# Second projection as one run of 36 matmuls behind the seven products, and the gates' sums over tokens on TensorE

## The chip, the cores and the metric

The kernel runs on one core of a Trainium2 chip. The metric is the device time of one execution in microseconds (us), lower is better. Engines are named PE (TensorE), DVE (VectorE), ACT (ScalarE), POOL (GpSimd) and SP (the queue that starts the loads); PEld is the load of PE's stationary operand.

## The reference

Chunked attention (2 x 8 heads, 768 tokens, head size 64) is followed by two mixtures of experts over 1536 tokens of 512 numbers: one with 4 experts and given gates, one with 8 experts whose gates are worked out from the first one's output by eight rounds of dividing by row sums and by column sums.

```python
def _moe_ref(x, domain_probs, w1, w2):
    p = domain_probs / (domain_probs.sum(-1, keepdims=True) + 1e-09)
    for e in range(E):                       # 4 experts
        h = np.maximum(x @ w1[e], 0.0)       # w1[e]: 512 x 1024
        out += p[:, e:e + 1] * (h @ w2[e])   # w2[e]: 1024 x 512

def _moe2_ref(x, w_gate, w1, w2):
    logits = x @ w_gate                      # 1536 x 8
    P = np.exp(logits - logits.max())
    for _ in range(8):
        P /= P.sum(1, keepdims=True) + 1e-09
        P /= P.sum(0, keepdims=True) + 1e-09  # over all 1536 tokens
        P *= N / E
    for e in range(E):                       # 8 experts
        out += P[:, e:e + 1] * (np.maximum(x @ w1[e], 0.0) @ w2[e])
```

## The kernel before

After the attention (the first 110 us) the work is 96 equal steps that the code calls quads: 24 jobs (an expert for one half of the tokens, 768) of four quads. The jobs stand in four passes of 4, 4, 8 and 8 jobs, so a new set of token operands begins at quads 16, 32 and 64 (called boundaries below). Every product of two fp32 matrices is made of three matmuls in the fp32r type, on a rounded high part and a low part that holds the rest (`in_three`, L438 to L441).

**First projection.** A quad makes four 128x384 blocks of the hidden layer from seven products (Winograd's form of a 2x2 block product). Product i (L443) is six matmuls of 384 columns. It accumulates in one of four PSUM banks, in the order `CHAIN = (0, 1, 0, 3, 0, 2, 3)`: products 2, 4 and 6 go on top of what is in a bank that ACT has first to copy away. So product 2 waits for `keep_part` 0, product 4 for `keep_part` 1 and product 6 for `keep_part` 2 (L453 to L460, L625). DVE then adds the kept parts to each block (`add`, L763), ACT makes the rounded hidden value (`hidden`, L630) and DVE its low part (`hidden`, L770).

**Second projection.** `down` (L467) multiplies two finished quads (a half of the hidden layer) by half of w2, for six token tiles; a tile is twelve matmuls of 512 columns. Quad q runs three tiles of the half before it, in twelve pieces of three matmuls that stand between the products as `PIECES = (2, 2, 1, 2, 2, 2, 1)` says. The first piece of an even quad waits for all hidden blocks of the quad just before it (L471). DVE adds a finished tile to the output rows (`accumulate`, L776).

**Weights.** SP loads w1 for a quad once `w1_raw` is free, which is when DVE's low part of the quad before is done (L245, `split_s` L747). POOL forms four sums (`sum_s`, L304), ACT rounds all seven stationary operands (`split_s`, L606), DVE takes the low part. w2 is rounded on ACT (L612) and its low part taken on DVE (`split_w2`, L752).

**Boundaries.** In the last quad of a pass ACT and DVE also make the seven token operands of the next pass (`next_tokens`, `split_t`, L618 and L758), and POOL forms sums of them (`sum_t` L314, `sum_t4` L334).

**Gates.** After the first mixture the output rows are transposed on PE (`turn_rows`, quads 18 and 33 to 34) and multiplied by `w_gate` (`logits`). From quad `SINK0` = 35 on DVE runs the eight rounds, three to a quad (`gates`, L820): row sums on DVE alone, column sums by DVE over a partition's tokens, then over the 128 partitions by POOL's `partition_all_reduce`. In POOL's queue these stand behind `sum_s(quad + 2)`:

```python
if quad + 2 < ALLQ:
    sum_s(quad + 2)
...
if SINK0 <= quad < SINK0 + 3:
    for it in range(3 * (quad - SINK0), min(3 * (quad - SINK0) + 3, SINKHORN)):
        pool.wait_ge(csum_ready, it + 1)
        pool.partition_all_reduce(ctotal, csum, P, RED.add).then_inc(ctotal_ready, 1)
```

No engine's queue is reordered: what stands behind a waiting instruction in the program text of its engine waits too.

## Time and profile before

| | |
|---|---|
| time, median of 3 runs | 1722.59 us (1720.34 to 1725.53) |
| profiled execution: its time | 1730.89 us |
| profiled execution: span | 1729.1 us |
| mean granted TensorE clock | 0.963 |
| PE busy | 1626.9 us, 94% of the span |
| DVE busy | 1003.6 us, 58% |
| ACT busy | 690.9 us, 40% |
| POOL busy | 329.8 us, 19% |

The span runs from the first to the last instruction of the profiled execution. PE's busy share counts overlapping matmuls as one, so how fast PE goes is read from the starts of successive matmuls. A granted clock of 1 is the full 2.4 GHz, 0.5 is the lower level of 1.2 GHz.

### The profile page before, as it was taken

Reading aid. Unit: us, or ns where it says so; the run is one execution under the profiler, and the core shown is the slowest. Engines: PE = TensorE matmul, PEld = TensorE weight load, DVE = VectorE, ACT = ScalarE, POOL = GpSimd, SP = SyncE. Lnnn points to the kernel's source line nnn. Section 1 sums busy time; section 2 is a strip of 40 time slices with the busy share of each in tenths; the row PEclk is TensorE's granted clock in tenths of the full one; section 3 lists DMA queues with packets and bytes.
Section 4 is the critical chain, followed back from the end, with each engine's and each line's share of the span. In section 5 each row is a group of like instructions: output and inputs, shape, how many; then the busy total and the mean of one; then the engine's idle time right before and its main releaser. Section 6 shows DMA issues by size and latency. Waiting matters only on the chain.

```text
span 1729.1 us, 21400 instructions
## 1 busy us (share of the span) xinstructions
PE 1626.9 (94%) x8673; PEld 1448.9 (84%) x8673; DVE 1003.6 (58%) x1445; ACT 690.9 (40%) x1058; POOL 329.8 (19%) x429
## 2 busy tenths in 40 slices
PE   6659999989999989759999999998999999999999
PEld 6648888879888879648888888887888888888887
DVE  5455655664565564536656565657565556556563
ACT  5443344443334443213444434434334443444441
POOL 2211113121111322011111111132111111111110
PEclk9779999999999999889999999999999999999999
DMA  9832122211212221111121222121222121121210
GB/s 161 127 67 85 62 62 72 62 49 49 86 61 62 73 61 49 40 46 49 61 73 62 61 86 62 49 85 49 97 85 61 50 86 61 56 79 62 78 57 37
DMA packets 158930, 117.75 MB, mean 68 GB/s; under 512 B 31336, under 2 KB 129640, under 8 KB 158832
## 3 DMA queue, kind: packets, MB, share of 16 engines
q1 hardware_dynamic: 158832, 116.39, 23.9%
q8 instruction: 68, 1.11, 0.3%
q14 instruction: 30, 0.25, 0.1%
HBM read 113.22 MB, written 3.15 MB: 67 GB/s over the span
## 4 chain that ended last, share of the span: by engine, by line
PE 85%; DVE 5%; SPq 3%; issue 2%; DMA 2%; ACT 1%; POOL 1%; POOLq 0%
PE banks L439 28%; PE banks L441 28%; PE banks L440 28%; SPq L229 1%; DVE t_lo L760 1%; DVE s_lo L749 1%; SPq L228 1%; DMA w_raw<-in_moe_w 1%; PE banks L497 1%; DVE banks L768 1%; ACT h_hi L632 1%; DMA v_bd<-in_mem_v 1%; DVE h_lo L772 1%; PE banks L425 0%; PE banks L489 0%
## 5 line engine op out<-in xcount | busy, mean ns | idle before, releaser
L439 PE MATMUL banks<-t_lo,s_hi 128*128 128x384 f32 x1344 | 459.6, 342 | 35.9 <-DVE h_lo L772 33.3
L439 PE MATMUL banks<-w_lo,h_hi 128*128 128x512 f32 x1152 | 459.7, 399 | 20.6 <-DVE h_lo L772 19.9
L440 PE MATMUL banks<-w_hi,h_hi 128*128 128x512 f32 x1152 | 459.5, 399 | 0.0
L441 PE MATMUL banks<-w_hi,h_lo 128*128 128x512 f32 x1152 | 458.7, 398 | 0.0
L441 PE MATMUL banks<-t_hi,s_lo 128*128 128x384 f32 x1344 | 456.9, 340 | 0.0
L440 PE MATMUL banks<-t_hi,s_hi 128*128 128x384 f32 x1344 | 454.5, 338 | 0.0
L768 DVE TENSOR_TENSOR banks<-banks,part 128x384 f32<-128x384 f32 x384 | 216.3, 563 | 362.7 <-PE banks L441 220.9
L632 ACT ACTIVATE h_hi<-banks 128x384 fp32r<-128x384 f32 x384 | 188.9, 492 | 555.3 <-DVE banks L768 555.3
L628 ACT ACTIVATE part<-banks 128x384 f32<-128x384 f32 x384 | 188.8, 492 | 392.8 <-PE banks L441 392.6
L439 PEld LDWEIGHTS banks<-t_lo,s_hi 128*128 128x128 f32 x1344 | 256.5, 191 | 67.1 <-issue 36.4
L772 DVE SCALAR_TENSOR_TENSOR h_lo<-banks,h_hi 128x384 fp32r<-128x384 f32 x384 | 213.4, 556 | 163.7 <-ACT h_hi L632 163.7
L307 POOL TENSOR_TENSOR w_raw<-w_raw 128x256 f32<-128x256 f32 x96 | 72.3, 753 | 1206.0 <-DMA w_raw<-in_moe_w 1206.0
L440 PEld LDWEIGHTS banks<-t_hi,s_hi 128*128 128x128 f32 x1344 | 256.1, 191 | 28.0
L439 PEld LDWEIGHTS banks<-w_lo,h_hi 128*128 128x128 f32 x1152 | 219.0, 190 | 59.3 <-DVE h_lo L772 35.8
L441 PEld LDWEIGHTS banks<-w_hi,h_lo 128*128 128x128 f32 x1152 | 218.5, 190 | 48.8
L441 PEld LDWEIGHTS banks<-t_hi,s_lo 128*128 128x128 f32 x1344 | 255.8, 190 | 0.0
L790 DVE SCALAR_TENSOR_TENSOR rows<-banks,gate,rows 128x512 f32<-128x512 f32 x258 | 192.3, 745 | 82.1 <-PE banks L441 82.1
L440 PEld LDWEIGHTS banks<-w_hi,h_hi 128*128 128x128 f32 x1152 | 218.8, 190 | 23.2
L749 DVE TENSOR_TENSOR s_lo<-w_raw,s_hi 128x1792 fp32r<-128x1792 f32 x96 | 193.5, 2016 | 0.0
L610 ACT ACTIVATE s_hi<-w_raw 128x1792 fp32r<-128x1792 f32 x96 | 162.6, 1694 | 2.1 <-POOL w_raw L312 2.1
L755 DVE TENSOR_TENSOR w_lo<-w_raw,w_hi 128x1024 fp32r<-128x1024 f32 x96 | 117.0, 1219 | 2.4 <-ACT w_hi L615 2.4
L615 ACT ACTIVATE w_hi<-w_raw 128x1024 fp32r<-128x1024 f32 x96 | 101.0, 1052 | 0.0
(87 smaller groups left out, 642.5 us busy)
## 6 DMA issues: line engine op xcount, KB each, us to landing
w_raw<-in_moe_w SPq DMA_DIRECT2D x192, 256.0 KB, 3.2
w_raw<-in_moe_w SPq DMA_DIRECT2D x48, 1024.0 KB, 7.0
v_bd<-in_v SPq DMA_DIRECT2D x16, 308.0 KB
w_raw<-in_q SPq DMA_DIRECT2D x8, 384.0 KB, 6.0
k_in<-in_k SPq DMA_DIRECT2D x8, 384.0 KB
out_x<-rows SPq DMA_DIRECT2D x12, 256.0 KB, 2.8
v_bd<-in_mem_v SPq DMA_DIRECT2D x16, 48.0 KB
v_bd<-in_v SPq DMA_DIRECT2D x16, 10.0 KB
```

The lines of the kernel that those rows point to most:

```text
L439: pe.matmul(out_, lhs_hi, rhs_lo, start=start, stop=False, skip_group_check=chained)
L440: pe.matmul(out_, lhs_hi, rhs_hi, start=False, stop=False, skip_group_check=chained)
L441: return pe.matmul(out_, lhs_lo, rhs_hi, start=False, stop=stop, skip_group_check=chained)
L610: act.activation(s_hi[quad % 2][:], w1_raw[:, 1:PRODUCTS + 1, :, :], ACT.Copy).then_inc(s_hi_ready, 1)
L615: act.activation(w2_hi[m % 2][:, 2 * j:2 * j + 2, :], w2_raw[:, 2 * j:2 * j + 2, :], ACT.Copy).then_inc(w2_hi_ready, 1)
L628: act.activation(part[:, j, :], c_ps[(0, 0, 3, 0)[j]], ACT.Copy).then_inc(part_copied, 1)
L632: act.activation(hidden_at(h_hi, quad, k), c_ps[BLOCKS[k][0]], ACT.Relu).then_inc(h_hi_ready, 1)
L749: dve.tensor_tensor(out=s_lo[quad % 2][:], in0=w1_raw[:, 1:PRODUCTS + 1, :, :], in1=s_hi[quad % 2][:].bitcast(F32), op=ALU.subtract).then_ ...
L755: dve.tensor_tensor(out=w2_lo[m % 2][:, fs, :], in0=w2_raw[:, fs, :], in1=w2_hi[m % 2][:, fs, :].bitcast(F32), op=ALU.subtract).then_inc(w ...
L768: dve.tensor_tensor(out=bank, in0=bank, in1=part[:, (0, 2, 3, 1)[k], :], op=ALU.add).then_inc(c_added, 1)
L772: dve.scalar_tensor_tensor(out=hidden_at(h_lo, quad, k), in0=c_ps[BLOCKS[k][0]], scalar=0.0, in1=hidden_at(h_hi, quad, k).bitcast(F32), op ...
L790: dve.scalar_tensor_tensor(out=dst, in0=got, scalar=by, in1=dst, op0=ALU.mult, op1=ALU.add).then_inc(y_taken, 1)
```

## The change

The second projection of a quad no longer stands between the products. All seven products run back to back, then the three token tiles as one run of 36 matmuls of 512 columns (`TILES_BEHIND = 3`). The queues of ACT and DVE are put in a matching order: parts, additions and hidden blocks first, then the splits of the next quad's weights, the remaining token operands, and the accumulation of tiles. DVE's low part of w2 moves to POOL, where `sum_s` is now issued one quad ahead instead of two. The sums over partitions move from POOL to PE: a 128x128 matrix of ones is the stationary operand, the total of each column lands on all partitions in PSUM, and DVE reads it there; the factor N/E is taken in the same DVE instruction, one fewer per round. The largest logit is found by a transpose on PE, a DVE maximum and a matmul that spreads it. The transposes of output rows, the logits and the rescaling of rows shift by a place or so.

```diff
-PIECES = (2, 2, 1, 2, 2, 2, 1)
+TILES_BEHIND = 3
...
+        ones = sb("ones", [P, P])
...
-            TURNS[LAST_A[0] + 2, t] = ("turn", 0, t)
-        TURNS[LAST_A[0] + 2, 6] = ("logits", 0, 0)
-        for t, (dq, i) in enumerate(((1, 0), (1, 1), (1, 2), (1, 4), (2, 0), (2, 1))):
-            TURNS[LAST_A[1] + dq, i] = ("turn", 1, t)
-        TURNS[LAST_A[1] + 2, 3] = ("logits", 1, 0)
+            TURNS[LAST_A[0] + 2, t + 1] = ("turn", 0, t)
+        TURNS[LAST_A[0] + 3, 1] = ("logits", 0, 0)
+        for t in range(ST):
+            TURNS[LAST_A[1] + 1 + t // 3, t % 3 + 1] = ("turn", 1, t)
+        TURNS[LAST_A[1] + 2, 4] = ("logits", 1, 0)
         SINK0 = LAST_A[1] + 3
+        COLUMN_SUMS = {}
+        for it in range(SINKHORN):
+            COLUMN_SUMS[SINK0 + it // 3, (4, 7, 9)[it % 3]] = it
+        RESCALE = SINK0 + 3
...
+            pool.memset(ones[:], 1.0).then_inc(ones_ready, 1)
...
-            sum_s(1)
+            def split_w2(m, j):
+                pool.wait_ge(w2_hi_ready, 2 * m + j + 1)
+                fs = slice(2 * j, 2 * j + 2)
+                pool.tensor_tensor(out=w2_lo[m % 2][:, fs, :], in0=w2_raw[:, fs, :],
+                                   in1=w2_hi[m % 2][:, fs, :].bitcast(F32), op=ALU.subtract).then_inc(w2_lo_ready, 1)
             for quad in range(ALLQ):
+                if quad + 1 < ALLQ:
+                    sum_s(quad + 1)
                 for p in range(1, PASSES):
                     if quad == QUADS * (FIRST[p] - 1):
                         sum_t(p)
                     if quad == QUADS * FIRST[p] - 1:
                         sum_t4(p)
-                if quad + 2 < ALLQ:
-                    sum_s(quad + 2)
-                if quad == SINK0 - 1:
-                    pool.wait_ge(lmax_ready, 1)
-                    pool.partition_all_reduce(gmax, lmax, P, RED.max).then_inc(gmax_ready, 1)
-                if SINK0 <= quad < SINK0 + 3:
-                    for it in range(3 * (quad - SINK0), min(3 * (quad - SINK0) + 3, SINKHORN)):
-                        pool.wait_ge(csum_ready, it + 1)
-                        pool.partition_all_reduce(ctotal, csum, P, RED.add).then_inc(ctotal_ready, 1)
+                split_w2(quad // 2, quad % 2)
...
-            def down(m, t, f):
+            def down(m, t):
 
                 y, par = m * ST + t, m % 2
-                if t == 0 and f == 0:
+                if t == 0:
                     pe.wait_ge(h_lo_ready, 8 * (m + 1))
                     pe.wait_ge(w2_lo_ready, 2 * (m + 1))
-                if f == 0 and y >= 3:
+                if y >= 3:
                     pe.wait_ge(y_taken, y - 2)
                 ts = slice(t * P, (t + 1) * P)
-                mm = in_three(y_ps[y % 3], h_hi[par][:, f, ts], h_lo[par][:, f, ts], w2_hi[par][:, f, :],
-                              w2_lo[par][:, f, :], f == 0, f == 3)
-                if f == 3:
-                    mm.then_inc(y_summed, 1)
+                for f in range(4):
+                    mm = in_three(y_ps[y % 3], h_hi[par][:, f, ts], h_lo[par][:, f, ts], w2_hi[par][:, f, :],
+                                  w2_lo[par][:, f, :], f == 0, f == 3)
+                mm.then_inc(y_summed, 1)
+            def turn_largest():
+                pe.wait_ge(lmax_ready, 1)
+                pe.transpose(x_ps[0:1, P:2 * P], lmax, ident[:]).then_inc(lmax_turned, 1)
+            def spread_largest():
+                pe.wait_ge(gmax_ready, 1)
+                pe.wait_ge(ones_ready, 1)
+                pe.matmul(x_ps[:, 2 * P:2 * P + 1], ones[0:1, :], gmax[0:1, :], start=True, stop=True).then_inc(gmax_spread, 1)
+            def column_sums(it):
+                pe.wait_ge(csum_ready, it + 1)
+                if it == 0:
+                    pe.wait_ge(ones_ready, 1)
+                pe.matmul(x_ps[:, 0:EB], ones[:], csum, start=True, stop=True).then_inc(ctotal_ready, 1)
...
                     product(quad, i)
-                    for _ in range(PIECES[i]):
-                        if m >= 0:
-                            down(m, piece // 4, piece % 4)
-                        piece += 1
+                for j in range(TILES_BEHIND):
+                    if quad == SINK0 - 1 and j == 0:
+                        turn_largest()
+                    if quad == SINK0 - 1 and j == 1:
+                        spread_largest()
+                    if (quad, PRODUCTS + j) in COLUMN_SUMS:
+                        column_sums(COLUMN_SUMS[quad, PRODUCTS + j])
+                    if m >= 0:
+                        down(m, TILES_BEHIND * (quad % 2) + j)
             for t in range(ST):
-                for f in range(4):
-                    down(ALLM - 1, t, f)
+                down(ALLM - 1, t)
...
-                take_turned(quad, 0)
                 keep_part(quad, 0)
                 next_tokens(quad, 0)
+                take_turned(quad, 1)
+                next_tokens(quad, 1)
+                take_turned(quad, 2)
+                hidden(quad, 0)
+                keep_part(quad, 1)
+                take_turned(quad, 3)
+                keep_part(quad, 2)
+                take_turned(quad, 4)
+                keep_part(quad, 3)
+                take_turned(quad, 5)
+                hidden(quad, 1)
+                take_turned(quad, 6)
+                hidden(quad, 2)
+                hidden(quad, 3)
                 if quad + 1 < ALLQ:
                     split_s(quad + 1)
-                take_turned(quad, 1)
-                next_tokens(quad, 1)
-                hidden(quad, 0)
-                take_turned(quad, 2)
-                keep_part(quad, 1)
-                next_tokens(quad, 2)
-                take_turned(quad, 3)
                 split_w2(quad // 2, quad % 2)
-                keep_part(quad, 2)
-                next_tokens(quad, 3)
-                take_turned(quad, 4)
-                keep_part(quad, 3)
-                next_tokens(quad, 4)
-                hidden(quad, 1)
-                take_turned(quad, 5)
-                hidden(quad, 2)
-                next_tokens(quad, 5)
-                hidden(quad, 3)
-                next_tokens(quad, 6)
+                for i in range(2, PRODUCTS):
+                    next_tokens(quad, i)
...
-            def split_w2(m, j):
-                dve.wait_ge(w2_hi_ready, 2 * m + j + 1)
-                fs = slice(2 * j, 2 * j + 2)
-                dve.tensor_tensor(out=w2_lo[m % 2][:, fs, :], in0=w2_raw[:, fs, :], in1=w2_hi[m % 2][:, fs, :].bitcast(F32),
-                                  op=ALU.subtract).then_inc(w2_lo_ready, 1)
...
-                then(dve.tensor_scalar(crec, ctotal, EPS, None, ALU.add))
+                then(dve.tensor_scalar(crec, x_ps[:, 0:EB], EPS, EB / N, ALU.add, ALU.mult))
                 then(dve.reciprocal(crec, crec))
-                then(dve.tensor_scalar(crec, crec, N / EB, None, ALU.mult))
...
-                m, t0 = quad // 2 - 1, 3 * (quad % 2)
-                if m >= 1 or quad == 3:
-                    accumulate((quad - 1) // 2 - 1, 3 * ((quad - 1) % 2) + 2)
-                if quad == SINK0 + 3:
+                m, t0 = quad // 2 - 1, TILES_BEHIND * (quad % 2)
+                if quad > 2:
+                    accumulate((quad - 1) // 2 - 1, TILES_BEHIND * ((quad - 1) % 2) + 2)
+                gates(quad, 0)
+                next_tokens(quad, 0)
+                add(quad, 0)
+                next_tokens(quad, 1)
+                hidden(quad, 0)
+                for i in (1, 4):
+                    if TURNS.get((quad, i), ("",))[0] == "logits":
+                        take_logits(TURNS[quad, i][1])
+                gates(quad, 1)
+                add(quad, 1)
+                add(quad, 2)
+                hidden(quad, 1)
+                add(quad, 3)
+                hidden(quad, 2)
+                hidden(quad, 3)
+                gates(quad, 2)
+                if quad == RESCALE:
                     dve.wait_ge(y_taken, (HALVES * FIRST[2] + 2) * ST)
                     for t in range(ST):
                         dve.tensor_scalar(rows[0][:, t, :], rows[0][:, t, :], gate[:, t, EA:EA + 1], None,
                                           ALU.mult).then_inc(rescaled, 1)
                     dve.wait_ge(rescaled, ST)
-                gates(quad, 0)
-                next_tokens(quad, 0)
-                add(quad, 0)
-                if m >= 0:
-                    accumulate(m, t0)
-                hidden(quad, 0)
-                next_tokens(quad, 1)
+                if quad == SINK0 - 1:
+                    dve.wait_ge(lmax_turned, 1)
+                    dve.tensor_reduce(gmax[0:1, :], x_ps[0:1, P:2 * P], AX.X, ALU.max).then_inc(gmax_ready, 1)
                 if quad + 1 < ALLQ:
                     split_s(quad + 1)
                 next_tokens(quad, 2)
-                split_w2(quad // 2, quad % 2)
+                if m >= 0:
+                    accumulate(m, t0)
+                if quad == SINK0 - 1:
+                    dve.wait_ge(gmax_spread, 1)
+                    dve.tensor_scalar(nmax, x_ps[:, 2 * P:2 * P + 1], -1.0, None, ALU.mult).then_inc(nmax_ready, 1)
                 next_tokens(quad, 3)
-                if (quad, 3) in TURNS and TURNS[quad, 3][0] == "logits":
-                    take_logits(TURNS[quad, 3][1])
-                gates(quad, 1)
-                add(quad, 1)
-                hidden(quad, 1)
                 if m >= 0:
                     accumulate(m, t0 + 1)
-                next_tokens(quad, 4)
-                add(quad, 2)
-                hidden(quad, 2)
-                next_tokens(quad, 5)
-                add(quad, 3)
-                hidden(quad, 3)
-                next_tokens(quad, 6)
-                if (quad, 6) in TURNS:
-                    take_logits(TURNS[quad, 6][1])
-                if quad == SINK0 - 1:
-                    dve.wait_ge(gmax_ready, 1)
-                    dve.tensor_scalar(nmax, gmax, -1.0, None, ALU.mult).then_inc(nmax_ready, 1)
-                gates(quad, 2)
+                for i in range(4, PRODUCTS):
+                    next_tokens(quad, i)
```

## Rows read from the trace of the kernel before

**Rows 1.** The page: engines' busy time; two groups; the loads of w1.

```profile
PE 1626.9 (94%) x8673; PEld 1448.9 (84%) x8673; DVE 1003.6 (58%) x1445; ACT 690.9 (40%) x1058; POOL 329.8 (19%) x429
...
L790 DVE SCALAR_TENSOR_TENSOR rows<-banks,gate,rows 128x512 f32<-128x512 f32 x258 | 192.3, 745 | 82.1 <-PE banks L441 82.1
...
L610 ACT ACTIVATE s_hi<-w_raw 128x1792 fp32r<-128x1792 f32 x96 | 162.6, 1694 | 2.1 <-POOL w_raw L312 2.1
...
w_raw<-in_moe_w SPq DMA_DIRECT2D x192, 256.0 KB, 3.2
```

**Rows 2.** Waits between 695 and 792 us (total us, times, longest).

```profile
DVE cols L813 <- POOL cols L372: 36.2, 3, 12.2
...
PE banks L439 <- DVE h_lo L772: 33.0, 5, 11.2
...
POOL cols L372 <- issue: 17.8, 3, 6.0
```

**Rows 3.** Timeline of DVE, the low parts of w1, one per quad (start, duration).

```profile
333.07 2.02 DVE L749 TENSOR_TENSOR s_lo<-w_raw,s_hi 128x1792 fp32r<-128x1792 f32 x1
...
372.03 2.02 DVE L749 TENSOR_TENSOR s_lo<-w_raw,s_hi 128x1792 fp32r<-128x1792 f32 x1
...
700.76 2.01 DVE L749 TENSOR_TENSOR s_lo<-w_raw,s_hi 128x1792 fp32r<-128x1792 f32 x1
...
805.71 2.02 DVE L749 TENSOR_TENSOR s_lo<-w_raw,s_hi 128x1792 fp32r<-128x1792 f32 x1
...
1121.88 2.01 DVE L749 TENSOR_TENSOR s_lo<-w_raw,s_hi 128x1792 fp32r<-128x1792 f32 x1
```

**Rows 4.** Timeline of PE after a stall in quad 36.

```profile
724.28 0.63 PE L440 MATMUL banks<-w_hi,h_hi 128*128 128x512 f32 x1
724.71 0.63 PE L441 MATMUL banks<-w_hi,h_lo 128*128 128x512 f32 x1
```

**Rows 5.** Timeline of PE, second-projection matmuls: a run of six; the last run, 72.

```profile
1616.87 0.39 PE L439 MATMUL banks<-w_lo,h_hi 128*128 128x512 f32 x1
...
1618.03 0.39 PE L441 MATMUL banks<-w_hi,h_lo 128*128 128x512 f32 x1
...
1709.23 0.50 PE L439 MATMUL banks<-w_lo,h_hi 128*128 128x512 f32 x1 [1.07 <-DVE h_lo L772]
...
1725.48 0.39 PE L441 MATMUL banks<-w_hi,h_lo 128*128 128x512 f32 x1
```

**Rows 6.** Timeline of PE and ACT in quad 0, which has no second projection.

```profile
113.92 0.36 PE L441 MATMUL banks<-t_hi,s_lo 128*128 128x384 f32 x1
...
115.51 0.49 ACT L628 ACTIVATE part<-banks 128x384 f32<-128x384 f32 x1
...
116.22 0.34 PE L439 MATMUL banks<-t_lo,s_hi 128*128 128x384 f32 x1
...
119.17 0.34 PE L441 MATMUL banks<-t_hi,s_lo 128*128 128x384 f32 x1
...
121.01 0.41 PE L439 MATMUL banks<-t_lo,s_hi 128*128 128x384 f32 x1 [1.50 <-DVE h_lo L772]
```

**Rows 7.** Timeline of PE, DVE and ACT where quad 91 ends and 92 begins.

```profile
1643.86 0.34 PE L441 MATMUL banks<-t_hi,s_lo 128*128 128x384 f32 x1
...
1644.23 0.57 DVE L768 TENSOR_TENSOR banks<-banks,part 128x384 f32<-128x384 f32 x1 [0.35 <-PE banks L441]
...
1644.83 0.49 ACT L632 ACTIVATE h_hi<-banks 128x384 fp32r<-128x384 f32 x1 [1.54 <-DVE banks L768]
...
1645.36 0.56 DVE L772 SCALAR_TENSOR_TENSOR h_lo<-banks,h_hi 128x384 fp32r<-128x384 f32 x1 [0.56 <-ACT h_hi L632]
...
1645.61 0.34 PE L441 MATMUL banks<-t_hi,s_lo 128*128 128x384 f32 x1
...
1645.97 0.50 PE L439 MATMUL banks<-w_lo,h_hi 128*128 128x512 f32 x1
...
1646.31 0.40 PE L440 MATMUL banks<-w_hi,h_hi 128*128 128x512 f32 x1
```

**Rows 8.** Timeline of POOL and DVE in quad 15, before the first boundary.

```profile
349.77 3.56 POOL L339 TENSOR_TENSOR rows<-rows,t_two 128x768 f32<-128x768 f32 x1 [8.04 <-DVE t_lo L760]
...
351.55 2.60 DVE L760 TENSOR_TENSOR t_lo<-t_two,t_hi 128x768 fp32r<-128x768 f32 x1
```

More of the change, by code:

```diff
@@ L11 @@
 AX = mybir.AxisListType
-RED = bass.bass_isa.ReduceOp
 CHUNK, LEFT, RIGHT = 32, 16, 8
@@ L113, in build @@
         sink = sb("sink", [P, TILES, EB])
-        cols = sb("cols", [P, 3 * EB])
+        cols = sb("cols", [P, 2 * EB])
         w2_hi0 = sb("w2_hi0", [P, 4, DM], F32R)
@@ L138, in build @@
         tok_sum = small[:, 24:36]
-        csum, ctotal, crec = cols[:, 0:EB], cols[:, EB:2 * EB], cols[:, 2 * EB:3 * EB]
+        csum, crec = cols[:, 0:EB], cols[:, EB:2 * EB]
         lmax, gmax, nmax = small[:, 48:49], small[:, 49:50], small[:, 50:51]
@@ L175, in build @@
         logits_summed, logits_taken = sem("logits_summed"), sem("logits_taken")
-        lmax_ready, gmax_ready, nmax_ready, sink_exp = sem("lmax_ready"), sem("gmax_ready"), sem("nmax_ready"), sem("sink_exp")
-        csum_ready, ctotal_ready = sem("csum_ready"), sem("ctotal_ready")
+        lmax_ready, lmax_turned, gmax_ready = sem("lmax_ready"), sem("lmax_turned"), sem("gmax_ready")
+        gmax_spread, nmax_ready, sink_exp = sem("gmax_spread"), sem("nmax_ready"), sem("sink_exp")
+        csum_ready, ctotal_ready, ones_ready = sem("csum_ready"), sem("ctotal_ready"), sem("ones_ready")
         rescaled, stored = sem("rescaled"), sem("stored")
@@ L529, in _ @@
                 m = quad // 2 - 1
-                piece = 12 * (quad % 2)
                 for i in range(PRODUCTS):
@@ L537, in _ @@
                             logits(b)
+                    if (quad, i) in COLUMN_SUMS:
+                        column_sums(COLUMN_SUMS[quad, i])
                     product(quad, i)
-                    for _ in range(PIECES[i]):
-                        if m >= 0:
-                            down(m, piece // 4, piece % 4)
-                        piece += 1
+                for j in range(TILES_BEHIND):
[7 more added lines that the diff above has]
+                        down(m, TILES_BEHIND * (quad % 2) + j)
             for t in range(ST):
-                for f in range(4):
-                    down(ALLM - 1, t, f)
+                down(ALLM - 1, t)
         def kt_windows(u, at):
```

## The prediction

> **What bounds the kernel now.** I read the page first, then the waits, then the starts of single instructions. PE is busy for 94% of the span [rows 1], so outside the start only two things count: how fast PE issues matmuls, and where it stands still. For the undisturbed pace I took the same DVE instruction in two quads: 805.71 to 1121.88 us is twenty quads, 15.81 us each [rows 3]. A quad is 42 matmuls of 384 columns and 36 of 512. The short ones start every 0.175 us (5.25 us over 30 intervals [rows 6]), the long ones every 0.232 us in a run of six (1.16 over 5 [rows 5]): 7.35 + 8.35 = 15.70. The rest is a small stall once in two quads, at the first piece of an even quad. The last hidden block's low part ends at 1645.92, the matmul starts at 1645.97 where 1645.785 was due, and the next start is 0.34 later instead of 0.23 [rows 7]: 0.3 us, 0.15 per quad. So DVE, ACT, POOL and the loads are hidden in a steady quad; only the pace of the two kinds of matmul and that stall can be changed.
>
> The large loss is the gates. From quad 35's split to quad 39's are 104.95 us [rows 3], where four plain quads take 63.2: 41.7 us too many. PE waits 33.0 us of it for hidden low parts, in 5 waits [rows 2]. Those are late because DVE stands in its queue in front of the column totals, 36.2 us in 3 waits, and POOL itself has 17.8 us of "issue" in 3 pieces of up to 6.0 before a partition sum starts. The others of the 41.7 are the slow clock after each stall: 512-column matmuls then start every 0.43 us [rows 4], the lower of the two clock levels, against 0.232.
>
> **The change part by part.** All times below are counted from the start of a quad's first product.
>
> *Gates.* Removed: all of POOL's partition sums, -41.7. What comes back: eight column sums, a transpose and a spreading matmul on PE. None is in the trace. Below they cost no less than a broken pace, 0.3 us as in [rows 7]; with one or two short matmuls 0.45. Ten of them: 4.5 us (3 to 6). DVE's round of some 2.1 us (an estimate: about nine small instructions at a quarter of a microsecond) now delays `add` 0, and ACT's part copy behind it, which product 4 waits for. The column sum stands on PE just before product 4 and covers part of it. I take 1.2 us in each of three quads, 3.5 (0 to 9). Net -33.7. Since PE never waits long, the clock stays up.
>
> *One run of 36.* The longest run of 512-column matmuls in the trace is the last one: 72 starts from 1709.23 to 1725.48, 71 intervals, 0.229 us each, its slow first one included [rows 5]. At that pace 36 take 8.24 instead of 8.35, -0.11 a quad. The stall of 0.15 a quad goes too: the run now begins after seven products, over 7 us behind the hidden blocks that it needs. A new quad is 15.59 - a little for the change of kind, I take -0.22 against 15.81. Over the 92 quads that have a second projection: -20 us (-14 if only the stall goes, -26 if the run settles faster than the row's mean).
>
> *Seven products without cover.* This is the danger. Product i's last matmul starts at 1.05i + 0.875, and DVE or ACT see it 0.37 later (1643.86 to 1644.23 [rows 7]). So `add` 0 starts at 2.30, ACT's hidden 0.60 later [rows 7] at 2.90 and ends at 3.39, the copy of part 1 ends at 3.88, and PE knows 0.05 later, 3.93. Product 4 starts at 4.20 and its weight load one pace earlier, at 4.03. That is 0.1 us to spare, and product 2 has as much. Quad 0 of the kernel before already runs its products like this: ACT copies at 115.51, ends at 116.00, and the matmul at 116.22 keeps the pace; 31 starts from 113.92 to 119.17 have no gap [rows 6]. So I charge nothing. Were the cover gone, each miss costs 0.3 us and its lateness.
>
> *Weights.* `split_s` moves behind the hidden blocks. The last product is done at 7.5, two more additions and hidden blocks bring DVE to 9.4; ACT rounds from 8.7 to 10.4 (1.69 [rows 1]) and DVE's low part ends at 12.5 (2.02 [rows 3]). The next quad needs it at 15.6: 3 us to spare. The w1 load then starts; 3.2 us to landing [rows 1] and POOL's sums end near 3.5 in the next quad, needed at 8.7. The low part of w2 on POOL starts at 12.5 and is ready near 15, needed 7 us later, and its next load has a whole quad less 5 us. SP's queue keeps its order. All hidden, 0 us.
>
> *POOL beside DVE.* At 349.77 POOL's 768-column subtraction took 3.56 us; it ended only 1.7 after DVE's low part had ended at 351.63, and then DVE's own next one took 2.60 [rows 8] where its width is worth about 0.95. The two waited for each other whole. The Trainium skill says it as a rule (SBUF — State Buffer, "Who interferes with whom"): a DVE instruction with two SBUF inputs and a GpSimd one that reads SBUF hold a shared port in turn, the later fully blocked. By that rule too, a w2 split on POOL (2.3 us for 1024 columns by the 1.7) can push work on DVE. In a steady quad DVE is first and only accumulations follow, which read PSUM: 0.
>
> *Boundaries.* Quads 14 to 16 take 38.96 us where two plain ones take 31.62: 7.3 now [rows 3], three times. In the new order five token splits stand behind `split_s` on DVE, from 13.4 on: five at 0.87, three accumulations at 0.745 [rows 1], 2.4 us of the w2 split and 4 x 0.7 of POOL's sums in between, ending near 24.4. `add` 0 of the next quad, ACT's hidden and the part copy follow to about 26.0, where product 4 was due at 21.0: 5 us of stall, 2.4 of slow clock, and 1.0 in the quad before: 8.4. I take +1 each, +3 (-9 if POOL's and DVE's work do not collide, +12 if each costs 4 more).
>
> *Start.* Quads 0 and 1 have no second projection to cover `split_s`. Quad 0's last matmul starts at 119.17; add, hidden, rounding and low part bring the next quad to 124.4 instead of 121.01 [rows 6], +3.4, and the same once more at most in quad 2, where the old kernel stalls too: +5 (3.4 to 6.8). Two SP waits and POOL's sum of quad 2 stand behind the same split and are inside this.
>
> *End.* The 1.07 us wait before the last 72 matmuls goes [rows 5]: -1.2. Turns and logits stay as much work as they were: 0.
>
> **Sum**: -33.7 - 20 + 3 + 5 - 1.2 = -46.9. The profiled execution took 1730.89, so 1684.0 by its own time. The median shown is 8.3 lower than that execution, so on the median 1722.59 - 46.9 = 1675.7.
>
> **Rivals.** (a) The long matmuls keep their old pace, or the saved stall turns up elsewhere: 10 to 20 us less gain, 1686 to 1696. For it: the last run has no other engine's work beside it. Chance 0.16. (b) The 0.1 us to spare is not there, and every quad stalls before products 2 and 4. At 0.3 each over 94 quads +56, 1732, slower. It decides from (46.9 + 5)/94 = 0.55 us per quad; at one place alone +28, 1704. For it: 0.1 us is less than the jitter that one added wait brings; against it quad 0. Chance 0.05 for both places (slower), 0.03 for a sum within the bound, 0.06 for one. (c) DVE and POOL do not block each other where it counts, contrary to [rows 8]: the boundaries gain instead, 1664. Here the skill's rule would speak against. Chance 0.08. (d) The gates' new chain (PE, DVE, PE, three times a quad) stalls product 4 and the next quad by 4 to 5 us instead of 1.2: about +12, 1688. Chance 0.10. The forecast has the rest, 0.52.
>
> A difference of 0.3% (5.2 us) is about what a measurement of this kernel can tell from none. Faster by more: 0.52 + 0.16 + 0.06 + 0.08 + 0.10 = 0.92, within 0.03, slower 0.05. The forecast's own terms reach from 1662 (run -26, boundaries -4 more, gates -4) to 1690; with (a), (c) and (d) the range is 1660 to 1702.
>
> **What would show it.** Right: the low parts of w1 15.5 to 15.6 us apart in plain quads; starts of 512-column matmuls 0.229 apart through the run; no wait of PE for part copies; quads 35 to 39 within 8 us of plain ones and the clock at 1.0 there; a 5 us wait of PE for a part copy in quads 16, 32 and 64. Wrong: PE waiting for `part` in every quad, DVE's low part of w1 or tokens stretched beside POOL in plain quads, or the granted clock falling where the column sums stand.

## The result and the profile after

The changed kernel takes 1657.26 us (median of 4 runs, 1654.19 to 1664.7), the kernel before beside it 1723.44: ratio 0.9624, 95% interval 0.9587 to 0.9661. Faster, as forecast, but by 66.2 us where 46.9 were predicted; 1675.7 was the forecast, and the time lies 2.7 us below the range. The profiled execution took 1659.28, its span is 1657.4. One execution of a later kernel, the profiled one of early_split, took 2636.82 us at a granted clock of 0.555; it is in no median here and its rows are not read.

The page of the changed kernel, the engines' busy time and one group of instructions, beside [rows 1]:

```profile
PE 1589.5 (96%) x8692; PEld 1441.1 (87%) x8692; DVE 903.0 (54%) x1342; ACT 684.7 (41%) x1058; POOL 647.1 (39%) x517
...
L368 POOL TENSOR_TENSOR w_lo<-w_raw,w_hi 128x1024 fp32r<-128x1024 f32 x96 | 317.3, 3305 | 751.9 <-ACT w_hi L643 751.9
```

DVE lost 100 us of work and POOL gained 317. Neither number is a term of the sum: what counts is where PE goes slower or stands. For that the low parts of w1 are the clock again, one per quad; "low part k" is the one that quad k needs. The timeline of DVE, changed kernel: low parts 15 and 17, 34, 36, 40, 42 and 62.

```profile
330.08 2.02 DVE L774 TENSOR_TENSOR s_lo<-w_raw,s_hi 128x1792 fp32r<-128x1792 f32 x1 [1.03 <-ACT s_hi L638]
...
367.54 2.03 DVE L774 TENSOR_TENSOR s_lo<-w_raw,s_hi 128x1792 fp32r<-128x1792 f32 x1 [1.03 <-ACT s_hi L638]
...
650.11 2.03 DVE L774 TENSOR_TENSOR s_lo<-w_raw,s_hi 128x1792 fp32r<-128x1792 f32 x1 [1.03 <-ACT s_hi L638]
...
693.17 2.02 DVE L774 TENSOR_TENSOR s_lo<-w_raw,s_hi 128x1792 fp32r<-128x1792 f32 x1
...
756.97 2.03 DVE L774 TENSOR_TENSOR s_lo<-w_raw,s_hi 128x1792 fp32r<-128x1792 f32 x1 [1.03 <-ACT s_hi L638]
...
787.96 2.03 DVE L774 TENSOR_TENSOR s_lo<-w_raw,s_hi 128x1792 fp32r<-128x1792 f32 x1 [1.03 <-ACT s_hi L638]
...
1097.96 2.03 DVE L774 TENSOR_TENSOR s_lo<-w_raw,s_hi 128x1792 fp32r<-128x1792 f32 x1 [1.03 <-ACT s_hi L638]
```

From 42 to 62 are twenty quads in 310.00 us: 15.50 each, where [rows 3] have 15.81. From 36 to 40 are 63.80 us, 1.8 more than four plain quads; [rows 3] have 41.7 more. From 34 to 36 are 43.06, 12.1 more than two plain quads (before 41.65, 10.0 more). From 15 to 17 are 37.46, 6.5 more (before 7.3).

The two groups of waits of PE from 104 to 1640 us, all 96 quads of the changed kernel (total us, times, longest):

```profile
PE banks L446 <- ACT part L656: 13.5, 8, 3.7
PE banks L446 <- DVE s_lo L774: 10.1, 3, 4.9
```

Of the 10.1, 9.9 are the start (quads 1 and 2); the 13.5 are mostly the three boundaries. Counted from the first matmul of a product (110.27 before, 104.00 after) to the end, 65.4 us are gone:

| | predicted | measured |
|---|---|---|
| gates, turns and logits (low parts 34 to 42, less eight plain quads) | -33.7 | -37.9 |
| plain pace, 92 quads | -20 | -28.5 (15.81 to 15.50) |
| three boundaries (low parts 15 to 17, 31 to 33, 63 to 65) | +3 | -1.2 |
| start, to quad 4 | +5 | +2.5 |
| quads 18 and 19, first turns | 0 | +0.3 |
| end | -1.2 | -1.3 |
| sum | -46.9 | -66.1 |

The rows come to 0.7 us more than the 65.4: the quads right behind the boundaries stand in none of them, and quad 33 for one is 0.44 us longer than before (low parts 33 to 34, 16.98 instead of 16.54) although its plain pace is faster. A low part can lead or lag its quad, so the first row was also counted on PE, from the first matmul of a quad to that of a later one: quads 35 to 39 take 41.5 us over the plain pace before and 3.2 after, -38.3, and quads 33 and 34, with the turns and logits of the second half, take 12.0 us over it instead of 10.6, +1.4.

The other 6.3 us between the two spans lie ahead of the first product, in the attention, whose code the change leaves as it is. The first low part of w1 starts at 90.01 in the profile before and at 83.96 after; in the kernels below it starts anywhere from 79.87 (early_both) to 88.53 (early_both_dve). So this difference is not put down to the change.

### The profile page after: what moved, and what is told of

The parts are those of the page before. It is cut to its first block, busy times and chain, and to the rows that moved or that the text cites. A ratio compares the mean times of both kernels' runs of the same rounds, so it can differ in the third digit from the quotient of the medians.

```text
span 1657.4 us, 21410 instructions
## 1 busy us (share of the span) xinstructions
PE 1589.5 (96%) x8692; PEld 1441.1 (87%) x8692; DVE 903.0 (54%) x1342; ACT 684.7 (41%) x1058; POOL 647.1 (39%) x517
## 4 chain that ended last, share of the span: by engine, by line
PE 88%; DVE 4%; SPq 4%; ACT 2%; issue 1%; DMA 1%; ACTq 0%; DVEq 0%
PE banks L446 29%; PE banks L448 29%; PE banks L447 29%; DVE t_lo L779 2%; SPq L236 1%; SPq L235 1%; DVE s_lo L774 1%; PE banks L520 1%; DVE banks L787 1%; DMA v_bd<-in_mem_v 1%; ACT s_hi L638 1%; ACT h_hi L660 0%; ACT part L656 0%; SPq L238 0%; DVE rows L809 0%
## 5 line engine op out<-in xcount | busy, mean ns | idle before, releaser
L368 POOL TENSOR_TENSOR w_lo<-w_raw,w_hi 128x1024 fp32r<-128x1024 f32 x96 | 317.3, 3305 | 751.9 <-ACT w_hi L643 751.9
L446 PE MATMUL banks<-t_lo,s_hi 128*128 128x384 f32 x1344 | 459.2, 342 | 24.5 <-ACT part L656 13.5
L446 PE MATMUL banks<-w_lo,h_hi 128*128 128x512 f32 x1152 | 449.8, 390 | 0.0
L447 PE MATMUL banks<-w_hi,h_hi 128*128 128x512 f32 x1152 | 449.3, 390 | 0.0
L448 PE MATMUL banks<-w_hi,h_lo 128*128 128x512 f32 x1152 | 448.9, 390 | 0.0
L787 DVE TENSOR_TENSOR banks<-banks,part 128x384 f32<-128x384 f32 x384 | 207.1, 561 | 326.0 <-ACT part L656 190.8
L447 PEld LDWEIGHTS banks<-w_hi,h_hi 128*128 128x128 f32 x1152 | 216.5, 188 | 41.5
```

The costliest lines, as they stand in the source:

```text
L368: pool.tensor_tensor(out=w2_lo[m % 2][:, fs, :], in0=w2_raw[:, fs, :], in1=w2_hi[m % 2][:, fs, :].bitcast(F32), op=ALU.subtract).then_inc( ...
L446: pe.matmul(out_, lhs_hi, rhs_lo, start=start, stop=False, skip_group_check=chained)
L447: pe.matmul(out_, lhs_hi, rhs_hi, start=False, stop=False, skip_group_check=chained)
L448: return pe.matmul(out_, lhs_lo, rhs_hi, start=False, stop=stop, skip_group_check=chained)
L787: dve.tensor_tensor(out=bank, in0=bank, in1=part[:, (0, 2, 3, 1)[k], :], op=ALU.add).then_inc(c_added, 1)
```

## The experiments

Two kernels do one half of the change each (run_alone, gates_pe), three vary a step that the sum rests on (w2_dve, part_late, early_split), five follow what these showed. Times are medians; `ratio` is against the kernel before on the same chip.

| kernel | us (lowest to highest) | ratio (95%) |
|---|---|---|
| run_alone | 1685.53 (1682.26 to 1691.66) | 0.9776 (0.9753 to 0.98) |
| gates_pe | 1688.3 (1687.14 to 1689.44) | 0.9788 (0.9775 to 0.9802) |
| w2_dve | 1650.57 (1649.88 to 1655.9) | 0.9575 (0.9559 to 0.9591) |
| part_late | 1680.04 (1679.32 to 1680.76) | 0.974 (0.9721 to 0.976) |
| early_split | 1645.99 (1644.06 to 1649.1) | 0.9546 (0.9522 to 0.957) |
| early_again, the same | 1645.35 (1642.08 to 1648.02) | 0.954 (0.9506 to 0.9573) |
| four_runs | 1686.18 (1683.15 to 1689.21) | 0.9777 (0.9745 to 0.9809) |
| two_runs | 1668.49 (1667.25 to 1669.74) | 0.9678 (0.9637 to 0.9718) |
| early_both | 1639.22 (1634.75 to 1641.84) | 0.9502 (0.948 to 0.9524) |
| early_both_dve | 1643.24 (1637.04 to 1643.7) | 0.9512 (0.9488 to 0.9536) |

### run_alone: the changed kernel with POOL's partition sums

```diff
+                if SINK0 <= quad < SINK0 + 3:
+                    for it in range(3 * (quad - SINK0), min(3 * (quad - SINK0) + 3, SINKHORN)):
+                        pool.wait_ge(csum_ready, it + 1)
+                        pool.partition_all_reduce(ctotal, csum, P, RED.add).then_inc(ctotal_ready, 1)
                 split_w2(quad // 2, quad % 2)
...
-                    if (quad, PRODUCTS + j) in COLUMN_SUMS:
-                        column_sums(COLUMN_SUMS[quad, PRODUCTS + j])
```

> The run of 36 behind the products, with the partition sums left on POOL. Theory (the two parts add up, the gates are worth about 37 us and the run about 29): plain quads 15.50 us, PE waits of some 30 us between quads 35 and 39 again, 1695 us (1688 to 1703). Rival: in the new order POOL reaches its sums earlier, because only one quad's sums of w1 stand ahead of them, so that most of the gates' stall goes without PE: 1665 to 1680.

The new order alone (with the low part of w2 on POOL) saves 38.9 us. The time, 1685.53, lies below the theory's range and above the rival's. Its plain quads take 15.50, as the theory had it, and in the gates DVE waits as before, against the rival, but PE less. The waits by DVE and by PE between 650 and 790 us and by POOL between 640 and 760 (total, times, longest):

```profile
DVE cols L832 <- POOL cols L386: 33.8, 3, 14.3
...
PE banks L454 <- DVE s_lo L774: 23.7, 4, 10.1
...
POOL cols L386 <- issue: 17.6, 3, 5.9
```

The first partition sum of a quad still costs POOL 5.9 us of "issue". But low parts 34 to 42 are 167.89 us apart, 43.9 above plain quads, where the kernel before has 51.7: 7.8 us of the same stall are gone although the sums are still POOL's. That the long matmuls, now behind the products, cover them is likely and was not tried by itself.

### gates_pe: the kernel before with the sums on PE

```diff
+        for it in range(SINKHORN):
+            COLUMN_SUMS[SINK0 + it // 3 + (it % 3 == 2), (2, 5, 1)[it % 3]] = it
...
-                        pool.partition_all_reduce(ctotal, csum, P, RED.add).then_inc(ctotal_ready, 1)
...
+                    if (quad, i) in COLUMN_SUMS:
+                        column_sums(COLUMN_SUMS[quad, i])
                     product(quad, i)
```

> The kernel before with nothing changed but the partition sums on PE (column sums ahead of products 2, 5 and, of the next quad, 1). Theory: the 41.7 us of quads 35 to 39 shrink to some 4, plain quads stay at 15.81 on average, 1686 us (1683 to 1690). Rival: without the new order of the queues the sums stand wrong, DVE waits for PE and PE for DVE: two or three us in each of three quads stay, 1692 to 1696.

It saves 36.2 us, within the theory's range, and low parts 34 to 42 are nearer by the same: 178.21 before, 141.96 here. Plain quads keep their 15.81. The waits of PE from 650 to 790 us are 1.3 and 1.0 us, where [rows 2] have 33.0:

```profile
PE banks L486 <- DVE small L927: 1.3, 1, 1.3
PE banks L493 <- DVE cols L829: 1.0, 2, 0.6
```

The halves save 38.9 and 36.2, 75.1 together, and the whole saves 66.2. Most of the 9 us counted twice is seen in low parts 34 to 42: 7.8 by the order and 36.2 by the sums, 37.9 by both.

### w2_dve: the low part of w2 back on DVE

```diff
@@ pool
-                split_w2(quad // 2, quad % 2)
@@ dve
                     split_s(quad + 1)
+                split_w2(quad // 2, quad % 2)
                 next_tokens(quad, 2)
```

> The changed kernel with the low part of w2 back on DVE, behind the low part of w1. Theory (DVE and POOL block each other only where tokens are split): plain quads stay 15.50; at the three boundaries DVE loses a wait of 2.3 us and gains 1.2 of work, so the stall there is about 1 us shorter each: 1654 us (1650 to 1658). Rival: POOL's move relieves DVE everywhere and the low part of w1 or the accumulations come too late without it: plain quads over 15.6, 1667 or more.

The ratio is 0.0049 lower than that of the changed kernel (8 us; the two intervals still overlap, by 0.0004, so the times alone do not decide). The profile says where it lies: low parts 15 to 17 are 35.22 us apart instead of 37.46, 2.2 us less, 2.1 and 1.8 at the other two boundaries (1 each was expected), and low parts 34 to 42 are 135.79 apart instead of 137.85: 8.2 us in all. Against that the first four quads take 1.8 us more in this profile (see the start, below). In the changed kernel, timeline of POOL and of DVE in quad 15:

```profile
347.69 3.31 POOL L368 TENSOR_TENSOR w_lo<-w_raw,w_hi 128x1024 fp32r<-128x1024 f32 x1 [5.34 <-ACT w_hi L643]
...
346.69 2.03 DVE L774 TENSOR_TENSOR s_lo<-w_raw,s_hi 128x1792 fp32r<-128x1792 f32 x1 [1.03 <-ACT s_hi L638]
348.63 3.18 DVE L779 TENSOR_TENSOR t_lo<-t_two,t_hi 128x768 fp32r<-128x768 f32 x1
...
352.40 0.94 DVE L779 TENSOR_TENSOR t_lo<-t_one,t_hi 128x768 fp32r<-128x768 f32 x1
...
353.92 3.75 DVE L779 TENSOR_TENSOR t_lo<-rows,t_hi 128x768 fp32r<-128x768 f32 x3
```

In w2_dve, timeline of DVE at the same place:

```profile
353.34 1.22 DVE L773 TENSOR_TENSOR w_lo<-w_raw,w_hi 128x1024 fp32r<-128x1024 f32 x1
354.47 0.95 DVE L778 TENSOR_TENSOR t_lo<-t_two,t_hi 128x768 fp32r<-128x768 f32 x1
```

POOL begins inside DVE's 2.03, ends 2.3 us after it, and DVE's token split takes 3.18 instead of 0.95. So giving the 1.22 us of work to POOL made DVE's next instruction 2.2 us longer, 1.0 more than it had saved. The Trainium skill has the rule (SBUF — State Buffer, "Who interferes with whom"): a DVE instruction with two SBUF inputs and a GpSimd one that reads SBUF contend for a shared port, and the one that comes second is blocked while the first lasts. These rows agree with it.

That the boundary is 2.2 us shorter too is not the same 2.2. Product 4 of quad 16, the place where PE stands for a part copy, waits 3.00 us in w2_dve and 3.64 in the changed kernel; with the shorter wait in the quad before (0.69 instead of 0.83) that is 0.8 us. The rest is PE's clock. Timeline of PE in w2_dve, and the window behind it (length, PE busy, granted clock, DMA share and rate):

```profile
363.92 0.41 PE L439 MATMUL banks<-t_lo,s_hi 128*128 128x384 f32 x1 [3.00 <-ACT part L649]
...
364.00:368.00 4.00, 4.00 (x22) 1.00 0.01 4
```

Behind the 3.64 us the changed kernel runs 4 us at a granted clock of 0.58 (rows in the section on the prediction). At the second boundary it is the same, full clock behind 3.04 us; at the third w2_dve has slow clock too, 4 us at 0.57, where the changed kernel has 4 at 0.50 and 4 more at 0.73.

### part_late: one more ACT copy ahead of part 1

```diff
                 hidden(quad, 0)
+                if quad == 0:
+                    act.wait_ge(ident_ready, 1)
+                act.activation(pad[:], ident[:].unsqueeze(1).to_broadcast([P, 3, P]), ACT.Copy)
                 keep_part(quad, 1)
```

> The changed kernel with one more ACT copy of 384 columns in each quad, right before the copy of part 1 that product 4 waits for; its output is not used. Theory (0.12 us to spare before product 4's weight load): the copy comes 0.37 us late against that, so each quad loses 0.25 to 0.55 us, plain quads 15.75 to 16.05, 1681 to 1709 us. Rival: the margin is larger than worked out, since PE issues from a queue that holds work; under 5 us.

The copy only adds work: +22.8 us, where 24 to 52 were expected. Twenty plain quads take 313.63, 15.68 each, +0.18 instead of the 0.25 to 0.55 expected; the rest of the 22.8 lies at the start and the boundaries. Here is how PE meets it (timelines of ACT, the load of the stationary operand, and PE in part_late):

```profile
1011.80 0.48 ACT L657 ACTIVATE part<-banks 128x384 f32<-128x384 f32 x1
...
1012.33 0.19 PEld L447 LDWEIGHTS banks<-t_lo,s_hi 128*128 128x128 f32 x1 [0.21 <-ACT part L657]
...
1012.11 0.34 PE L449 MATMUL banks<-t_hi,s_lo 128*128 128x384 f32 x1
1012.33 0.44 PE L447 MATMUL banks<-t_lo,s_hi 128*128 128x384 f32 x1
1012.62 0.34 PE L448 MATMUL banks<-t_hi,s_hi 128*128 128x384 f32 x1
```

The load starts 0.05 after the copy's end, as the prediction had it, and in the same moment as its matmul. The pace breaks for two intervals: 0.22 and 0.29 instead of 0.17 each, so the matmul is 0.05 late and the next one 0.12 more. The same place in the changed kernel:

```profile
1013.48 0.49 ACT L656 ACTIVATE part<-banks 128x384 f32<-128x384 f32 x1
...
1014.15 0.19 PEld L446 LDWEIGHTS banks<-t_lo,s_hi 128*128 128x128 f32 x1
```

The copy ends at 1013.97 and the load is due at 1014.15. With the 0.05 from copy to load that leaves 0.13 us to spare, and it held in every plain quad.

### early_split and early_again: the split of w1 a quad earlier

```diff
-                if quad + 1 < ALLQ:
-                    split_s(quad + 1)
+                if quad + 2 < ALLQ:
+                    split_s(quad + 2)
```

(on ACT and on DVE; `sum_s` on POOL likewise; `split_s(1)` stands in the attention's last unit.)

> The changed kernel with the stationary operands of the first projection split one quad earlier (the sums of w1 two quads ahead again), so that nothing waits for them in quads 0 and 1. Theory (the start's cost is the unhidden split): the two waits of PE for the low part of w1, 4.9 us each, and the slow clock behind them, some 2.4 each, go; 2 to 4 us of ACT's queue come in; plain quads stay 15.50; 1646 us (1643 to 1651). Rival: the load of w1 and POOL's sums are the limit of these quads, as their chain of 10.5 us is longer than 7.3 us of products: under 4 us gained, 1653 to 1657.

> The same kernel as early_split, for a profile of it. Theory: plain quads 15.50, the start without PE's two waits of 4.9 for the low parts of w1 in quads 1 and 2, boundaries near those of the changed kernel; 1647 again, within 3.

early_again is the same kernel once more, for its rows. The ratios are 0.9546 and 0.954: 13 to 14 us less than the changed kernel (11 to 12 by the medians). In early_again the start is 4.5 us shorter (low parts 0 to 6 stand 86.61 apart, 102.1 with the one quad by which they are early, against 106.63), PE's waits for low parts of w1 are gone (5.1 us for part copies come instead), and a boundary exceeds plain quads by 4.0 instead of 6.5 (low parts 15 to 19, which are now split two quads ahead). So the time came as forecast and the mechanism only in part: the start gave less than half of what was expected, the three boundaries the larger share, which the expectations left as they were. Product 4 of quad 16 waits 2.55 us there and the granted clock stays at 1.00 behind it.

### four_runs and two_runs: the 36 matmuls cut up

```diff
+BEHIND = (0, 0, 0, 2, 2, 2, 6)
...
                     product(quad, i)
+                    for _ in range(BEHIND[i]):
+                        if m >= 0:
+                            down(m, 3 * (quad % 2) + piece // 4, piece % 4)
+                        piece += 1
```

(on top of early_split; four_runs is shown, two_runs has `BEHIND = (0, 0, 0, 6, 0, 0, 6)`. The number says how many pieces follow each product; a piece is three matmuls.)

> As early_split, with the 36 matmuls of a quad in four runs instead of one: six behind each of products 3, 4 and 5, eighteen behind product 6; same work, same queues of DVE and ACT. Theory (the long matmuls are slower only near the start of a run, about 0.028 us a run): plain quads 15.58, the pace of 512-column matmuls about 0.230 us, 8 us more than early_split. Rival: the faster pace came with the new order of the other engines or with w2's split on POOL, and not with the run: plain quads 15.50.

> The 36 long matmuls of a quad stand as two runs of eighteen, behind product 3 and behind product 6 (early weight split as in early_split). Theory 'each change of kind costs a fixed bit': before has six more changes than one run and a plain quad without its stall of 15.67, after has 15.50, so 0.17 over 6 = 0.03 per extra run; a plain quad here then takes 15.53. Rival 'a run pays at its start and only runs longer than some dozen matmuls reach 0.227': two of eighteen would cost about 0.1, 15.60 or more. In both, the second and third column sum of quads 35 to 37 now stand with no long matmul between them, so the gates' quads must be worse than with one run by the DVE rounds, 10 to 25 us in all; the time is 1660 to 1690.

Plain quads (low parts 42 to 62 and 70 to 94): one run 15.50, two runs 15.57 and 15.56, four runs 15.68 and 15.63. The means of four_runs hold a few quads of 16.3 to 16.5; nearly all others take 15.60 between PE's starts, those of two_runs 15.56. The kernel before, seven runs, takes 15.67 in the quads without its stall. More changes of kind, a slower quad, but two runs cost more than the fixed 0.03 of the one theory and less than the 0.10 of the other. The starts show why. Timeline of PE in two_runs, the first, sixth and last start of a run of eighteen:

```profile
893.36 0.39 PE L449 MATMUL banks<-w_lo,h_hi 128*128 128x512 f32 x1
...
894.52 0.39 PE L451 MATMUL banks<-w_hi,h_lo 128*128 128x512 f32 x1
...
897.24 0.40 PE L451 MATMUL banks<-w_hi,h_lo 128*128 128x512 f32 x1
```

The first five intervals take 1.16 us, 0.232 each, to the hundredth what [rows 5] show for a run of six; the twelve behind them take 2.72, 0.2267. The run of 36 in the changed kernel, and the 42 short matmuls behind it, first, sixth and last start:

```profile
1001.95 0.39 PE L446 MATMUL banks<-w_lo,h_hi 128*128 128x512 f32 x1
...
1003.10 0.39 PE L448 MATMUL banks<-w_hi,h_lo 128*128 128x512 f32 x1
...
1009.90 0.40 PE L448 MATMUL banks<-w_hi,h_lo 128*128 128x512 f32 x1
1010.14 0.34 PE L446 MATMUL banks<-t_lo,s_hi 128*128 128x384 f32 x1
...
1011.02 0.34 PE L448 MATMUL banks<-t_hi,s_lo 128*128 128x384 f32 x1
...
1017.27 0.34 PE L448 MATMUL banks<-t_hi,s_lo 128*128 128x384 f32 x1
```

Long: 1.15 over the first five, then 6.80 over 30, 0.2267. Short: 0.88 over five, 0.176, then 6.25 over 36, 0.1736. So a run of either kind is slower over its first six matmuls, by 0.01 to 0.03 us a run, and one of only six never reaches its pace. On the mean of 42 plain quads the short matmuls take 7.31 us in one run and 7.34 in two, the long ones 8.19 and 8.22.

The whole times are worse than that (two_runs +23 us against early_again, four_runs +40 against early_split, by the medians; for four_runs 8 were expected) for another reason: the third column sum of a quad now has no long matmul before it, and PE waits for DVE's round. The column sums in two_runs, second and third of quad 35:

```profile
694.64 0.29 PE L505 MATMUL banks<-cols,ones 128*128 128x8 f32 x2
...
698.71 0.39 PE L505 MATMUL banks<-cols,ones 128*128 128x8 f32 x2 [3.78 <-DVE cols L836]
```

Low parts 34 to 40 are 129.20 us apart there, 110.97 in early_again. The same eight sums cost 2.7 us in the changed kernel's quads 35 to 37 (counted on PE's starts, over the plain pace) only because each stands behind work that covers DVE's round. The two times, 1668.49 and 1686.18, hold this share, so they say little about the pace; the plain quads do.

### early_both and early_both_dve: token splits ahead of weight splits too

```diff
@@ dve (on top of early_split; on act the same, with split_w2 behind split_s)
-                if quad + 2 < ALLQ:
-                    split_s(quad + 2)
-                next_tokens(quad, 2)
+                for i in range(2, PRODUCTS):
+                    next_tokens(quad, i)
+                if quad + 2 < ALLQ:
+                    split_s(quad + 2)
```

(The first two token splits of a pass's last quad also move, behind the first hidden block.)

> As early_split, and in the last quad of a pass all token operands are split ahead of the weights, the first two behind the first hidden block. Theory (at a boundary product 4 waits because five token splits stand between it and add 0): the waits of PE for a part copy in quads 16, 32 and 64, 3.6 us each, those of 0.6 to 0.8 in the quads before, and the slow clock go; of 20.4 us in all some 3 stay; 1629 us (1626 to 1637). Rival: DVE and POOL are then still blocking each other and the stall only moves to the next load of w1: half of it stays, 1637 or more.

> As early_both, with w2's low part on DVE. Theory (w2 on POOL costs only where DVE's token splits meet it): nearly nothing is left to meet, so the same as early_both within 2 us. Rival: POOL's 3.3 us instruction also costs in the quads of the gates, where DVE's own small instructions have two SBUF inputs: 3 to 5 us faster than early_both.

early_both is the fastest: 0.9502, some 21 us below the changed kernel by the ratios (18 by the medians), 6 of them against early_again (whose interval it overlaps). It was expected at 1629 and came at 1639.22, in the rival's range: PE still waits 8.7 us for part copies, in 9 pieces of up to 2.2, between 100 and 1640 us. A boundary now exceeds plain quads by 2.4 us (low parts 15 to 19, timeline of DVE in early_both, 64.39 less 62.0):

```profile
305.20 2.02 DVE L778 TENSOR_TENSOR s_lo<-w_raw,s_hi 128x1792 fp32r<-128x1792 f32 x1 [1.03 <-ACT s_hi L640]
...
369.59 2.03 DVE L778 TENSOR_TENSOR s_lo<-w_raw,s_hi 128x1792 fp32r<-128x1792 f32 x1 [1.03 <-ACT s_hi L640]
```

Putting w2's low part back on DVE gains nothing any more (0.9512, the intervals overlap): the tokens that it had blocked now stand ahead of it.

## Why the prediction was right in kind and short in size

**Gates, -33.7, measured -37.9.** The mechanism was right: gates_pe alone takes 36.2 us, and run_alone still shows DVE's wait of 33.8 us. The granted clock is 1.00 from 682 to 760 us, as forecast. Eight us were to come back. On PE's starts 3.2 did, so two terms were too large. Ten PE steps were charged 4.5 us at 0.3 to 0.45 each. The row of a column sum (timeline of PE, changed kernel):

```profile
685.43 0.33 PE L448 MATMUL banks<-t_hi,s_lo 128*128 128x384 f32 x1
685.61 0.28 PE L502 MATMUL banks<-cols,ones 128*128 128x8 f32 x2
685.74 0.42 PE L446 MATMUL banks<-t_lo,s_hi 128*128 128x384 f32 x1
686.00 0.34 PE L447 MATMUL banks<-t_hi,s_hi 128*128 128x384 f32 x1
```

From 685.43 to 686.00 are 0.57 us where two intervals of 0.174 stood: 0.22 a sum. And the 3.5 us for product 4 behind DVE's round came to 0.5. These are PE's waits between 695 and 760 us, the second of them for a low part of w1:

```profile
PE banks L446 <- ACT part L656: 0.5, 2, 0.3
PE banks L446 <- DVE s_lo L774: 0.2, 1, 0.2
```

The 2.1 us guessed for a round was right (685.92 to 687.96), and the column sum on PE covered it. Rival (d), 4 to 5 us of it in each of three quads, is refuted. The term that failed the other way is "turns and logits, 0": quads 33 and 34 lost 1.4 us. In w2_dve they lost nothing and in early_again 3.0, and what sets this was not tried.

**One run of 36, -20, measured -28.5.** This is the step that failed, by its size and not by its mechanism, and the largest share of the miss. Its -0.22 a quad was 0.15 for the stall and 0.07 for the pace. Quads of the kernel before without the stall take 15.67, the others 15.95, all of the changed kernel 15.50: 0.14 for the stall, 0.17 for the pace. The text took 0.229 from the mean over 72 matmuls, which contains their slow first starts, gave 0.04 of it back "for the change of kind", and gave the short matmuls no gain at all; settled, the runs showed 0.2267 and 0.1736. The case was named in the text ("-26 if the run settles faster than the row's mean"), but not chosen, and its 26 is short too. (The quads with a second projection are 94, not 92; counted from quad 4 on, as in the table, they are 92.) Rival (a), that the pace stays, is refuted by run_alone's 15.50.

**Products without cover, 0, held.** 0.1 to 0.2 us was enough in every plain quad, and part_late shows the cliff right behind it: +0.18 a quad for one copy of 0.42. Rival (b)'s price, 0.3 a miss and its lateness, was too high for the one miss tried.

**Boundaries, +3, measured -1.2.** The place and the kind of wait were right: PE stands at product 4 of quad 16 for the part copy, but 3.64 us instead of 5, and the clock then costs less than the 2.4 charged. The timeline of PE and the windows around it (length, PE busy, granted clock, DMA share and rate):

```profile
359.86 0.41 PE L446 MATMUL banks<-t_lo,s_hi 128*128 128x384 f32 x1 [3.64 <-ACT part L656]
...
356.00:360.00 4.00, 0.36 (x3) 1.00 0.00 0
360.00:364.00 4.00, 4.00 (x15) 0.58 0.01 4
364.00:368.00 4.00, 4.00 (x19) 0.99 0.00 0
```

At 0.58 for 4 us the loss is an estimated 1.7. That it is lost at all hangs on a little: behind the 3.00 us of w2_dve the clock stayed up. Also mis-sized was the blocking between POOL and DVE: 5.2 us of it were put on DVE's path (2.4 for the w2 split, 2.8 for the sums), and the rows above show 2.2 and 0.9 (3.75 for three token splits of 0.95). The sum itself was added wrong in the other direction: 13.4 and its terms make 25.2, not 24.4, so a correct sum had forecast 0.8 more of stall. The block was real, rival (c) is refuted by the 3.18, but POOL's sums paid for most of theirs themselves: they take 1.32 to 1.56 us each there, and 0.72 to 0.76 where DVE leaves them alone (run_alone, from 685.24).

**Start, +5, measured +2.5.** PE waits 4.9 us twice for low parts of w1, at the places named, and early_split takes both away. The first was sized right: quad 0 takes 14.20 us from its first matmul to that of quad 1, 10.74 before, +3.5 for the +3.4 charged. Quad 1 adds 2.7 more, but quad 2 then takes 17.01 where the kernel before, which stalls there, has 20.44. In the whole stretch PE waits 9.9 us now and 6.6 before (4.9 for hidden low parts, 1.7 for part copies), 3.3 more. The prediction named that stall ("where the old kernel stalls too") and gave it too little. And part of the +2.5 is luck of one execution. The stretch takes 60.76 us in this profile and 62.56 and 62.57 in run_alone and w2_dve, whose start has the same waits of 4.9; that would be +4.3. The difference is the clock. Windows on quad 1, changed kernel and run_alone:

```profile
118.00:132.00 14.00, 9.13 (x42) 0.88 0.14 39
...
117.50:132.90 15.40, 10.36 (x43) 0.72 0.12 36
```

**What is open.** Why a run of matmuls is slow at its start was not tried, nor what sets how deep and how long the clock falls after a stall. The four largest misses all fell on the same side (4.2 + 8.5 + 4.2 + 2.5); nothing here says that they have one cause.

## What to carry to other kernels

When PE is 94% busy, read its pace by position within a run of equal matmuls, not as a mean: here 0.17 us a quad, a few nanoseconds a matmul, made 16 us; only the gates' stall was worth more to this change. Where a slow engine's answer is fetched through PE, place the fetch so that long matmuls stand between two of them; by that alone the same sums cost some 2 us (early_again) or some 18 (two_runs). And before giving an idle GpSimd work that reads SBUF, look at what VectorE does beside it: 1.2 us taken off DVE made its next instruction 2.2 longer at the place where DVE was late.

## What the runs showed of the hardware beyond this

- The first six matmuls of a run start 0.232 us apart for 512 columns and 0.176 for 384, the later ones 0.2267 and 0.1736, at a granted clock of 1.
- At the first boundary a stall of PE of 3.64 us was followed by 4 us at a granted clock of 0.58 (changed kernel), one of 3.00 us (w2_dve) and one of 2.55 (early_again) by full clock. At the third boundary 3.01 us were followed by 4 us at 0.57 (w2_dve), so the length of the stall alone does not decide it.
- A stationary load that came late and let its matmul start 0.05 us late cost PE 0.17 us in all, spread over two intervals (part_late).
- The first partition sum of each quad cost POOL 5.8 to 5.9 us before it began, the second of the same quad nothing of the kind; the first subtraction behind the sums began after 7.2 to 8.2 us of "issue" (run_alone).
